# Evening out the token blocks of a fused attention and feed-forward kernel: 416/448/448/416 columns become four of 432

## What is computed

```python
def _moe_ref(x, w_gate, w_val, w_out):          # 512 -> 1536 -> 512
    g = x @ w_gate
    silu = g * (1.0 / (1.0 + np.exp(-g)))
    val = x @ w_val
    return (silu * val @ w_out).astype(np.float32)

def _moe2_ref(x, w_in, w_out, alpha):           # 512 -> 2048 -> 512
    h = x @ w_in
    g = np.maximum(h, 0.0) + alpha * np.minimum(h, 0.0)
    return (g @ w_out).astype(np.float32)

attn_out = _attn_ref(**attn_kwargs)             # (4, 8, 576, 64)
x = np.ascontiguousarray(attn_out.transpose(0, 2, 1, 3)).reshape(B * S, H * D)
x = _moe_ref(x=x, **moe_kwargs)
return _moe2_ref(x=x, **moe2_kwargs)
```

## Time and profile before

| | us |
|---|---|
| median of 3 runs | 951.43 |
| lowest and highest | 951.32 and 952.82 |
| the run that was profiled, device time | 952.82 |
| its span, from first to last instruction | 951.0 |
| PE busy in the span | 932.0 (98%) |
| DVE busy | 504.7 (53%) |
| ACT busy | 280.1 (29%) |
| POOL busy | 140.9 (15%) |
| granted TensorE clock, mean | 0.998 of full |

### The profile page before, as it was taken

The page is one execution under the profiler, slowest core; times in us unless marked ns, Lnnn a source line. Parts: engine busy times, 40 slices in busy tenths (PEclk is TensorE's granted clock), DMA queues, the critical chain, the costliest instruction groups (busy, mean ns, idle before and its releaser), DMA issues.

```text
span 951.0 us, 19243 instructions
## 1 busy us (share of the span) xinstructions
PE 932.0 (98%) x7944; PEld 859.5 (90%) x7944; DVE 504.7 (53%) x996; ACT 280.1 (29%) x707; POOL 140.9 (15%) x167
## 2 busy tenths in 40 slices
PE   4899999999999999999999999999999999999998
PEld 3899999999998888898999999999999999999997
DVE  8899777544466665554323345444444444444443
ACT  5566444322233433222224422111111111111111
POOL 7876011000011000000026620000000000000000
PEclk9999999999999999999999999999999999999999
DMA  9763322311122221300053320020100100200000
GB/s 282 232 197 110 105 82 88 98 50 41 41 69 80 81 81 49 98 22 14 1 172 110 123 92 1 1 67 1 35 32 1 67 1 1 67 1 1 34 1 34
DMA packets 31077, 63.24 MB, mean 66 GB/s; under 512 B 3344, under 2 KB 13584, under 8 KB 30992
## 3 DMA queue, kind: packets, MB, share of 16 engines
q1 hardware_dynamic: 30992, 62.02, 20.5%
HBM read 52.57 MB, written 9.44 MB: 65 GB/s over the span
## 4 chain that ended last, share of the span: by engine, by line
PE 95%; DVE 1%; DMA 1%; ACT 1%; SPq 1%; issue 0%; POOL 0%; DVEq 0%; ACTq 0%
PE ps L1087 53%; PE ps L1132 21%; PE ps L1115 16%; PE ps L1035 2%; PE ps L971 1%; DMA vsrc_early<-vsrc 1%; PE ps L981 1%; PE ps L1048 1%; PE ps L1019 1%; DVE h_lo L909 1%; SPq L364 0%; PE ps L1096 0%; ACT turned_early L599 0%; SPq L357 0%; SPq L368 0%
## 5 line engine op out<-in xcount | busy, mean ns | idle before, releaser
L669 ACT CAST h_hi<-hidden 128x384 fp32r<-128x384 f32 (+3 forms) x168 | 86.3, 514 | 416.6 <-DVE hidden L942 329.3
L1087 PE MATMUL ps<-x_hi,w_hi 128*128 128x416 f32 (+2 forms) x573 | 199.2, 348 | 0.0
L1087 PE MATMUL ps<-x_lo,w_hi 128*128 128x416 f32 (+2 forms) x573 | 193.2, 337 | 0.0
L1087 PE MATMUL ps<-x_hi,w_lo 128*128 128x416 f32 (+2 forms) x573 | 193.2, 337 | 0.0
L909 DVE TENSOR_TENSOR h_lo<-hidden,h_hi 128x384 fp32r<-128x384 f32 (+3 forms) x168 | 108.0, 643 | 72.3 <-ACT h_hi L669 72.3
L940 DVE TENSOR_SCALAR gated<-ps,alpha_sb 128x384 f32<-128x384 f32 x96 | 59.3, 618 | 158.5 <-PE ps L1087 158.5
L1132 PE MATMUL ps<-w_hi,h_hi 128*128 128x512 f32 x288 | 112.3, 390 | 0.5 <-DVE h_lo L909 0.5
L1132 PE MATMUL ps<-w_hi,h_lo 128*128 128x512 f32 x288 | 112.6, 391 | 0.0
L1087 PEld LDWEIGHTS ps<-x_hi,w_hi 128*128 128x128 f32 x573 | 108.0, 188 | 5.1 <-issue 0.2
L1132 PE MATMUL ps<-w_lo,h_hi 128*128 128x512 f32 x288 | 112.4, 390 | 0.0
L1087 PEld LDWEIGHTS ps<-x_hi,w_lo 128*128 128x128 f32 x573 | 107.8, 188 | 3.2
(11 more groups left out here) (140 smaller groups left out, 1471.5 us busy)
## 6 DMA issues: line engine op xcount, KB each, us to landing
w_home<-w SPq DMA_DIRECT2D x68, 256.0 KB, 3.9
qk<-qk SPq DMA_DIRECT2D x30, 436.0 KB, 3.7
vsrc_one<-vsrc SPq DMA_DIRECT2D x58, 144.0 KB
vwin<-vwin SPq DMA_DIRECT2D x30, 192.0 KB, 2.4
x_raw<-y_t SPq DMA_DIRECT2D x6, 768.0 KB, 5.9
out<-y_sb SPq DMA_DIRECT2D x5, 768.0 KB, 4.0
y_t<-y_sb SPq DMA_DIRECT2D x2, 896.0 KB, 4.7
y_t<-y_sb SPq DMA_DIRECT2D x2, 832.0 KB, 4.4
```

Source lines behind the costliest of these rows:

```text
L669: nc.scalar.copy(h_hi[r][:, 0:width], hidden[r][:, 0:width]).then_inc(h_hi_ready, 1)
L1087: mm = nc.tensor.matmul(out_ps, w[:, piece, 128 * k:128 * k + 128], x_parts[low][:, k, :], start=(k == 0 and n == 0), stop=(k == KC - 1 an ...
```

## The change

Blocks 2 to 5 of the first layer become equally wide: 432 columns each, in place of 416, 448, 448 and 416. `STARTS`, `HOMES` and the ring's length follow (1008 columns in place of 1024), and so do the tiles that are as wide as the widest block. The places of the attention units are as before.

Half-batch 3 (tokens 864 to 1151) is now shared evenly by blocks 2 and 3, which don't lie side by side in the ring: 144 columns go to 288 and 144 to 576. ACT's rounding and DVE's low part of that half-batch write two runs of 144 columns in place of one of 288, through `x_at` and `x_from`. The pad ahead of `x2_hi_odd` is gone.

```diff
-SPANS = (288, 288, 416, 448, 448, 416)
-STARTS = (0, 288, 576, 992, 1440, 1888)
-HOMES = (448, 736, 160, 576, 0, 448)
-HALVES_AT = (448, 736, 160, 448, 736, 0, 288, 576)
-RING, WIDEST = 1024, max(SPANS)
+SPANS = (288, 288, 432, 432, 432, 432)
+STARTS = (0, 288, 576, 1008, 1440, 1872)
+HOMES = (432, 720, 0, 576, 0, 432)
+RING, WIDEST = 1008, max(SPANS)
@@
-            sb("odd_start", [128, 16], where=second_x)
@@ def x_at(ring, k, a):
-            return ring[:, k, HALVES_AT[a]:HALVES_AT[a] + TB]
+            if a == 3:
+                return ring[:, k, TB:3 * TB].rearrange("p (n s) -> p n s", n=2)[:, :, 0:TB // 2]
+            first = (432, 720, 0, None, 720, 0, 288, 576)[a]
+            return ring[:, k, first:first + TB]
+
+        def x_from(tile, a):
+
+            return tile[:, :].rearrange("p (n s) -> p n s", n=2) if a == 3 else tile[:, :]
@@ def split_x_hi(a, k, mode):
-                nc.scalar.copy(x_at(x_hi, k, a), x_f32[mode][k][:, :]).then_inc(x_hi_ready, 1)
+                nc.scalar.copy(x_at(x_hi, k, a), x_from(x_f32[mode][k], a)).then_inc(x_hi_ready, 1)
@@ def split_x_lo(a, k, mode):
-                nc.vector.tensor_tensor(x_at(x_lo, k, a), x_f32[mode][k][:, :], x_at(x_hi, k, a).bitcast(F32), ALU.subtract).then_inc(x_lo_ready, 1)
+                nc.vector.tensor_tensor(x_at(x_lo, k, a), x_from(x_f32[mode][k], a), x_at(x_hi, k, a).bitcast(F32), ALU.subtract).then_inc(x_lo_ready, 1)
```

## The result

| | before | after |
|---|---|---|
| median, us | 951.38 | 958.64 |
| lowest and highest | 950.76 to 952.82 | 957.58 to 960.65 |
| ratio, 95% interval | | 1.0077 [1.0056, 1.0097] |
| profiled run, device time | 952.82 | 959.2 |
| its span | 951.0 | 957.4 |

What follows compares the result with a forecast made beforehand. PE was taken as the bound, its time a sum of matmul distances. Blocks 5, 2, 4 and 3 gave +3.4 + 3.0 - 3.0 - 3.0 = +0.4 us, so 951.43 became 951.8 us; range 949.0 to 956.5.

Steps and rivals of the forecast that it cites:

- What bounds the kernel: Blocks 2 to 5: PE waits for no other engine, so their 373.6 us are a sum of distances between matmul starts.
- The price of 432 columns: Blocks 2 to 5: 194.6 ns a matmul, midway between 186.7 at 416 and 202.5 at 448 columns.
- rival 2: Blocks 2 to 5: 432 is as bad a width as 448; +1.4 to +2.1 us, 952.8 to 953.5; chance 0.18.
- Rival 1: Blocks 2 to 5: 432 is a good width, surplus 13.3 ns; -0.6 to -2.2 us, 949.2 to 950.8; chance 0.24.
- rival 3: Blocks 2 to 5: the distance jumps at 432, to 200.0 ns; +8.5 us, 959.9; chance 0.12.
- Why 448 was the odd one out: At 448 columns a matmul leaves 15.8 or 20.0 ns over N/2.4; the other widths leave 12.5 to 14.4.
- A fixed surplus: Distance as N/2.4 plus a constant: said to hold for 384 and 416, not 448; otherwise -0.6 to -2.2 us.
- low bound: Blocks 2 to 5: 432 columns at 193.3 ns; sum -2.2 us on settled distances, -0.6 on block times.
- The covers: Attention units and block starts: turned probabilities keep 0.55 us, `x_lo` 1.1 ahead of block 4; no wait of PE.
- Edits at nothing: Elementwise work, two-run writes, stores of y, new start addresses of ring slices and second-layer operands: no cost.
- Rival 5: Slices' new start addresses cost something: 0.5 ns on 2592 matmuls is +1.3 us, 1 ns +2.6; chance 0.03.
- The range: Whole kernel: 949.0 to 956.5 us, taking in a jump in half of the stretches.

## Why the prediction was wrong, point by point

- **What bounds the kernel**: right. PE waits for no one after block 2, before and after the change, and the time is a sum of distances from matmul to matmul.
- **The price of 432 columns**, taken midway at 194.6 ns: a little low. Settled pieces show 195.4, which is nearer to rival 2's 195.8. That the sum came out is partly luck: it went midway between two prices, and that of 448 was set by where its operands lay, not by its width. With 448 at its better distance the same widths cost 2.2 us. In the sum the slip mattered little: each block time came within 0.4 us of the forecast, and the four together at 374.2 for 374.1. Rival 1 falls, rival 2 has the better single price and a sum 0.8 us too high, and the jump to 200 ns that rival 3 feared for a width that is no multiple of 32 didn't come. That the measured 958.64 lies near rival 3's 959.9 is chance: its jump was to be in the first layer. Its limit of 195.5 ns was also too low; by the prediction's own sums, +1.9 us is passed at 195.7 ns on settled distances and at 196.1 on block times.
- **Why 448 was the odd one out**: the prediction left that open and should not have. Its 15.8 to 20 ns were no property of the width. The runs with the ring and with the h tiles moved took the surplus to 13.7 and 14.1 in exactly the lines whose operand moved, and the run with both moved took it to 13.3. Had I asked why one of five widths breaks the pattern, the start addresses would have come up.
- **A fixed surplus**: the prediction said that by a fixed surplus the change would give its low bound. A surplus that is the same at every width leaves no change at all, since as many columns are gained as lost; the low bound holds for 13.3 ns at 432 with 15.8 left at 448. The formula of the Trainium skill that it drew on ("TensorE: Matmul & The Clock Gate", section Back-to-back issue gap) is given there for a matmul issued by itself, not for pairs of load and matmul as here.
- **The covers**: right. No wait of PE on the turned probabilities or on `x_lo`; DVE's low part of 288 columns takes 0.44 to 0.46 us throughout, in two runs of 144 as in one.
- **Edits at nothing**: this is the step that failed. It put the second layer's new start addresses at 0 us, and they cost 6.6. It said that second-layer operands run at the common surplus of 13.3 ns while lying off 128 bytes, and took this as a sign that an address costs nothing. The row showed only that the address of that day was a good one. The change took the tiles away from it, and a price can't be read from a row in which it isn't paid. And the step named the x tiles alone; the h tiles, whose four starts drifted apart when they became 16 columns narrower, weren't in it.
- **Rival 5**, start addresses, named the mechanism and had a chance of 0.03. Its price was put on the 2592 matmuls of the first layer at 0.5 to 1 ns. It fell on the 2016 of the second, at some 3 ns for 384 columns (2.11 or 2.12 for 2.08) and 3 to 6 for 512 (2.08 or 2.10 for 2.05). The test that the prediction proposed for it, second-layer pieces off 2.08 and 2.05, is what found it.
- **The range** ended at 956.5, 2.1 us short of the measured 958.64, since it took rival 3 for the only long tail.

## What to carry to other kernels

When a tile's width changes in a kernel that lays its memory out in a row, everything behind it moves, and where TensorE is the bound, a shift of 64 bytes can cost more than the edit is about: compare the start addresses of all TensorE operands, modulo 256 bytes, before and after. An unexplained pad may be the tuning, and taking it out is a change of its own. A curve with one point off it is a question to settle before one interpolates through it.

## What the runs showed of the hardware

With a weight load for every matmul in float32, the distance between matmuls depends on how the moving operand's start lies to the stationary one's, modulo 256 bytes: 173.3 to 176.7 ns at 384 columns, 226.7 to 233.3 at 512, 200.0 to 206.7 at 448. Moving everything together by 64 bytes changes nothing (952.08 us against 952.33). The best distance differs by width, and I have no rule for it: of those tried, 64 bytes for 384 and 448, 0 for 512, 0 or -64 for 416, hardly any difference for 432. The shortest surplus over N/2.4 found is 13.3 ns for 384, 416, 448 and 512 columns alike (for 512 it is the 2.04 us for nine in the run with the x2 tiles at other remainders), and 15.0 for 432.

A matmul's own operands don't settle its pace alone. With the pad gone, 512-column matmuls slowed from 2.05 to 2.08 us for nine while only the operand of the 384-column ones had moved, and those were back at 173.3 ns by the time the nine began. So a rhythm is carried from one shape to the next.

The Trainium skill ("TensorE: Matmul & The Clock Gate", section Step-by-step: what each phase is for) says that the moving operand and the weight load have independent read ports, so that loading the next weights takes no read bandwidth from the running matmul. No run here measures the bandwidth, but the two are not without effect on one another: moving one of them by 64 bytes changes the pace by some 1 to 2.5%, moving both doesn't. Whether the two reads meet in the memory, or whether it is the turn-taking of loads and matmuls that falls into another rhythm, stays open.
